# Attention scores in blocks of 128 rows, in parts of three and two blocks, in place of six blocks of 96

## The reference

```python
def _attn_ref(q, k, v):                       # (8, 8, 576, 64): batch, head, row, dim
    k_p = k.reshape(B, H, Sp, 8, D).mean(axis=3)    # 72 keys in place of 576
    v_p = v.reshape(B, H, Sp, 8, D).mean(axis=3)
    scores = scale * np.matmul(q, k_p.transpose(0, 1, 3, 2))
    scores = scores - np.max(scores, axis=-1, keepdims=True)
    attn = np.exp(scores)
    attn = attn / (np.sum(attn, axis=-1, keepdims=True) + 1e-09)
    return np.matmul(attn, v_p).astype(np.float32)

x = attn_out.transpose(0, 2, 1, 3).reshape(4608, 512)
h = x @ w_in;  x = np.maximum(0.01 * h, h) @ w_out          # layer 1, (512, 2048), (2048, 512)
h = x @ w2_in; x = h * np.clip(h + 3, 0, 6) / 6 @ w2_out    # layer 2, same sizes
```

## Time and profile before

| | |
|---|---|
| time, median of 3 runs | 1733.42 us (1729.87 to 1739.12) |
| the profiled execution's own time | 1732.34 us |
| its span in the trace | 1730.6 us |
| mean granted TensorE clock | 0.992 of full |
| instructions | 33189 |
| PE, DVE, ACT, POOL busy | 98%, 59%, 37%, 23% of the span |
| moved by DMA | 366.83 MB, 212 GB/s mean |

### The profile page before, as it was taken

The page is one execution under the profiler, slowest core; times in us unless marked ns, Lnnn a source line. Parts: engine busy times, 40 slices in busy tenths (PEclk is TensorE's granted clock), DMA queues, the critical chain, the costliest instruction groups (busy, mean ns, idle before and its releaser), DMA issues. The chain is left out here.

```text
span 1730.6 us, 33189 instructions
## 1 busy us (share of the span) xinstructions
PE 1691.3 (98%) x10588; PEld 1506.7 (87%) x10588; DVE 1024.0 (59%) x1807; ACT 632.5 (37%) x1329; POOL 394.1 (23%) x427
## 2 busy tenths in 40 slices
PE   7999999999999999999999999999999999999999
PEld 6788888988888888899999888989898888989898
DVE  7767776686766867666454655454544444444444
ACT  4554443333333433333222333333333333333332
POOL 6226542021120212103332202121211112121200
PEclk8999999999999999999999999999999999999999
DMA  7756877667676676767777757575757675757562
GB/s 199 228 159 201 271 249 247 214 201 259 204 243 220 208 247 215 242 196 268 239 258 245 257 172 224 176 220 175 218 170 220 178 219 171 223 173 223 173 197 77
DMA packets 215810, 366.83 MB, mean 212 GB/s; under 512 B 22464, under 2 KB 47040, under 8 KB 215744
## 3 DMA queue, kind: packets, MB, share of 16 engines
q1 hardware_dynamic: 215744, 366.04, 67.3%
HBM read 308.28 MB, written 57.67 MB: 211 GB/s over the span
## 5 line engine op out<-in xcount | busy, mean ns | idle before, releaser
L1416 PE MATMUL ps_h<-xs_hi,ring 128*128 128x256 f32 x3808 | 823.8, 285 | 20.5 <-ACT p L1045 15.9
L1416 PEld LDWEIGHTS ps_h<-xs_hi,ring 128*128 128x128 f32 x3808 | 645.5, 190 | 69.5 <-ACT p L1045 19.8
L1416 PE MATMUL ps_h<-xs_lo,ring 128*128 128x256 f32 x1904 | 537.4, 282 | 0.0
L1416 PEld LDWEIGHTS ps_h<-xs_lo,ring 128*128 128x128 f32 x1904 | 361.2, 190 | 27.0
L931 ACT ACTIVATE g_hi<-gate 128x512 fp32r<-128x512 f32 x288 | 181.9, 632 | 404.6 <-DVE gate L1126 221.8
L1185 DVE TENSOR_TENSOR u<-ps_h,p 128x256 f32<-128x256 f32 x272 | 114.2, 420 | 205.9 <-PE ps_h L1416 155.0
L1369 PE MATMUL ps_y<-g_hi,wout_hi 128*128 128x512 f32 x576 | 229.2, 398 | 0.5 <-DVE y_stage L1181 0.3
L1370 PE MATMUL ps_y<-g_lo,wout_hi 128*128 128x512 f32 x576 | 228.7, 397 | 0.0
L1370 PE MATMUL ps_y<-wout_lo,g_hi 128*128 128x512 f32 x576 | 227.8, 395 | 0.0
L1369 PE MATMUL ps_y<-wout_hi,g_hi 128*128 128x512 f32 x576 | 227.5, 395 | 0.1
L1371 PE MATMUL ps_y<-g_hi,wout_lo 128*128 128x512 f32 x576 | 226.1, 393 | 0.0
(11 more groups left out here) (115 smaller groups left out, 2021.4 us busy)
## 6 DMA issues: line engine op xcount, KB each, us to landing
ring<-w_in_split SPq DMA_DIRECT2D x920, 256.0 KB, 2.8
w_in_split<-ring SPq DMA_DIRECT2D x56, 256.0 KB, 3.6
w_in_split<-stage SPq DMA_DIRECT2D x56, 256.0 KB, 4.3
k_raw<-in_kT SPq DMA_DIRECT2D x32, 288.0 KB, 3.4
q_raw<-in_qT SPq DMA_DIRECT2D x32, 288.0 KB, 3.1
v_raw<-in_v SPq DMA_DIRECT2D x32, 288.0 KB
x0T<-x_stage SPq DMA_DIRECT2D x32, 288.0 KB, 4.4
x1T<-y_stage SPq DMA_DIRECT2D x36, 256.0 KB, 3.8
```

The costliest lines, as they stand in the source:

```text
L1416: mm = pe.matmul(banks[BANK_OF[r]], a, b[:, r, c, :], start=r in OPENS and c == 0 and n == 0, stop=c == 1 and n == 2, skip_group_check=True)
```

## The change

The six blocks of 96 rows become five of 128. The first part has the blocks at rows 0, 128 and 256; the second those at 384 and 448. The last two overlap by 64 rows, which are scored and normalized again; of the last block only its rows 64 to 127 are transposed (`AGAIN`). So a unit has 5 score matmuls (weights 128 x 128), passes of 128 partitions x 432 and 128 x 288 on DVE and ACT, 10 transposes (8 of 128 rows and 2 of 64), and products of 384 columns in `pv0` and of 192 in `pv1`. `units[0]` gets two buffers for q, used by turns, and its q load waits for the scores of the unit before the last. The x0 loads of tiles 1 to 6 move from places 18, 30 and 42 to 20, 32 and 44, those of tile 0 likewise by two, and the loads of tile 0 come one or two places earlier. `gap` is resized so that later buffers keep their places. The diff, with context and like edits left out:

```diff
@@ -15,10 +15,13 @@
-ROWS = 96
-SUB = S // ROWS
-HALF_SUB = SUB // 2
-HALF = S // 2
+BLOCK_AT = ((0, P, 2 * P), (3 * P, S - P))
+PART_BEGINS = (0, 3 * P)
+PART_QUERIES = (3 * P, S - 3 * P)
+SLOTS = (slice(0, 6), slice(6, 10))
+AGAIN = 4 * P - (S - P)
@@ -49,15 +52,15 @@
-X_PLACES = (18, 30, 42, 53)
+X_PLACES = (20, 32, 44, 53)
-FIRST_LOAD_PLACES = (6, 19, 30, 41)
+FIRST_LOAD_PLACES = (4, 18, 29, 40)
-FIRST_X_PLACES = (22, 33, 44, 54)
+FIRST_X_PLACES = (24, 35, 46, 54)
@@ -159,22 +162,23 @@
-            u.q_raw = buf("q_raw", [P, 2, HALF])
+            u.q_raw = [buf(f"q_raw{i}_", [P, S]) for i in range(1 if c else 2)]
-                buf("gap", [P, 4 * HALF + PAIR_KEYS])
+                buf("gap", [P, 2 * S + PAIR_KEYS - 240])
-            u.prob = buf("prob", [ROWS, 2, HALF_SUB * 2, KEYS])
-            u.row_max = buf("row_max", [ROWS, 2, HALF_SUB * 2])
-            u.pT_hi = buf("pT_hi", [KEYS, 2, HALF], F32R)
-            u.x0_stage = buf("x0_stage", [P, 2, HALF])
+            u.prob = buf("prob", [P, 10, KEYS])
+            u.row_max = buf("row_max", [P, 12])
+            u.pT_hi = buf("pT_hi", [KEYS, 2, PART_QUERIES[0]], F32R)
+            u.x0_stage = buf("x0_stage", [P, S])
...
@@ -229,6 +233,9 @@
+        def q_of(b, c):
+            return buffers(b, c).q_raw[0 if first(b) else c % 2]
@@ -382,8 +389,10 @@
-                above_zero(sp, scores_done, 2 * freed(b, c))
-                sp.dma_start(u.q_raw[:], qT[b, c]).then_inc(q_loaded[c], 16)
+                if not first(b):
+                    sp.wait_ge(scores_done, 2 * (freed(b, c) - 1))
+                sp.dma_start(q_of(b, c)[:], qT[b, c]).then_inc(q_loaded[c], 16)
@@ -534,7 +542,7 @@
-            sp.dma_start(units[0].q_raw[:], qT[1, 0]).then_inc(q_loaded[0], 16)
+            sp.dma_start(q_of(1, 0)[:], qT[1, 0]).then_inc(q_loaded[0], 16)
@@ -955,13 +963,14 @@
-                        nc.scalar.activation(u.prob[:, half], u.prob[:, half], ACT.Exp,
-                                             scale=SCORE_SCALE).then_inc(exp_ready, 1)
+                        nc.scalar.activation(u.prob[:, SLOTS[half]], u.prob[:, SLOTS[half]],
+                                             ACT.Exp, scale=SCORE_SCALE).then_inc(exp_ready, 1)
-                    nc.scalar.activation(u.pT_hi[:], u.ps[0:KEYS, :, 0:HALF], ACT.Copy
+                    n_q = PART_QUERIES[half]
+                    nc.scalar.activation(u.pT_hi[:, :, 0:n_q], u.ps[0:KEYS, :, 0:n_q], ACT.Copy
@@ -969,8 +978,10 @@
-                    nc.scalar.activation(u.x0_stage[:, half, :], u.ps[:, half, 0:HALF],
-                                         ACT.Copy, scale=V_SCALE).then_inc(x0_copied, 1)
+                    begins, n_q = PART_BEGINS[half], PART_QUERIES[half]
+                    nc.scalar.activation(u.x0_stage[:, begins:begins + n_q],
+                                         u.ps[:, half, 0:n_q], ACT.Copy, scale=V_SCALE
+                                         ).then_inc(x0_copied, 1)
@@ -1206,34 +1218,37 @@
-                        nc.vector.tensor_reduce(u.row_max[:, half], scores(u, half), AXIS_X,
+                        nc.vector.tensor_reduce(u.row_max[:, SLOTS[half]], scores(u, half), AXIS_X,
-                        nc.vector.tensor_tensor(u.prob[:, half], scores(u, half),
-                                                spread(u.row_max[:, half]), ALU.subtract
+                        nc.vector.tensor_tensor(u.prob[:, SLOTS[half]], scores(u, half),
+                                                spread(u.row_max, half), ALU.subtract
-                        nc.vector.tensor_reduce(u.row_sum[:, half], u.prob[:, half], AXIS_X,
-                                                ALU.add).then_inc(sum_ready, 1)
...
-                    dve.wait_ge(pT_hi_ready, 2 * n + int(name[-1]) + 1)
-                    nc.vector.tensor_tensor(u.pT_lo[:], u.ps[0:KEYS, :, 0:HALF],
-                                            u.pT_hi[:].bitcast(F32), ALU.subtract
+                    half = int(name[-1])
+                    n_q = PART_QUERIES[half]
+                    dve.wait_ge(pT_hi_ready, 2 * n + half + 1)
+                    nc.vector.tensor_tensor(u.pT_lo[:, :, 0:n_q], u.ps[0:KEYS, :, 0:n_q],
+                                            u.pT_hi[:, :, 0:n_q].bitcast(F32), ALU.subtract
@@ -1449,10 +1464,10 @@
-                        for at in range(HALF_SUB):
+                        for at, begins in enumerate(BLOCK_AT[half]):
-                                u.ps[0:ROWS, half, at * PAIR_KEYS:(at + 1) * PAIR_KEYS],
-                                u.q_raw[:, half, at * ROWS:(at + 1) * ROWS], u.kT[:],
+                                u.ps[:, half, at * PAIR_KEYS:(at + 1) * PAIR_KEYS],
+                                q_of(b, c)[:, begins:begins + P], u.kT[:],
@@ -1461,10 +1476,13 @@
-                        for j in range(HALF_SUB):
-                            mm = pe.transpose(u.ps[0:KEYS, hd, j * ROWS:(j + 1) * ROWS],
-                                              u.prob[:, half, 2 * j + hd, :],
-                                              ident[0:ROWS, 0:ROWS])
+                        for j, begins in enumerate(BLOCK_AT[half]):
+                            rows = slice(AGAIN if begins == S - P else 0, P)
+                            to = begins + rows.start - PART_BEGINS[half]
+                            mm = pe.transpose(
+                                u.ps[0:KEYS, hd, to:to + P - rows.start],
+                                u.prob[rows, SLOTS[half].start + 2 * j + hd, :],
+                                ident[rows, rows])
@@ -1472,8 +1490,10 @@
-                        mm = product(u.ps[:, half, 0:HALF], (u.v_hi[:, hd, :], u.v_lo[:, hd, :]),
-                                     (u.pT_hi[:, hd, :], u.pT_lo[:, hd, :]), hd == 0, hd == 1)
+                        n_q = PART_QUERIES[half]
+                        mm = product(u.ps[:, half, 0:n_q], (u.v_hi[:, hd, :], u.v_lo[:, hd, :]),
+                                     (u.pT_hi[:, hd, 0:n_q], u.pT_lo[:, hd, 0:n_q]),
+                                     hd == 0, hd == 1)
```

More of the change, by code:

```diff
@@ L166, in attention_buffers @@
             if c:
-                buf("gap", [P, 4 * HALF + PAIR_KEYS])
+                buf("gap", [P, 2 * S + PAIR_KEYS - 240])
             u.v_hi = buf("v_hi", [KEYS, 2, P], F32R)
             u.v_lo = buf("v_lo", [KEYS, 2, P], F32R)
-            u.prob = buf("prob", [ROWS, 2, HALF_SUB * 2, KEYS])
-            u.row_max = buf("row_max", [ROWS, 2, HALF_SUB * 2])
-            u.row_sum = buf("row_sum", [ROWS, 2, HALF_SUB * 2])
-            u.row_den = buf("row_den", [ROWS, 2, HALF_SUB * 2])
-            u.row_inv = buf("row_inv", [ROWS, 2, HALF_SUB * 2])
-            u.pT_hi = buf("pT_hi", [KEYS, 2, HALF], F32R)
-            u.pT_lo = buf("pT_lo", [KEYS, 2, HALF], F32R)
-            u.x0_stage = buf("x0_stage", [P, 2, HALF])
+            u.prob = buf("prob", [P, 10, KEYS])
+            u.row_max = buf("row_max", [P, 12])
+            u.row_sum = buf("row_sum", [P, 12])
+            u.row_den = buf("row_den", [P, 12])
+            u.row_inv = buf("row_inv", [P, 12])
+            u.pT_hi = buf("pT_hi", [KEYS, 2, PART_QUERIES[0]], F32R)
+            u.pT_lo = buf("pT_lo", [KEYS, 2, PART_QUERIES[0]], F32R)
+            u.x0_stage = buf("x0_stage", [P, S])
             return u
@@ L324, in first_chunk @@
         def first_chunk(c):
-            return units[c].x0_stage[:].rearrange("p a n -> p (a n)")[:, 0:N]
+            return units[c].x0_stage[:, 0:N]
         def ring_slot(q):
@@ L398, in store_x0 @@
                 sp.dma_start(x0T[c * P:(c + 1) * P, bass.ds(b * S, S)],
-                             buffers(b, c).x0_stage[:].rearrange("p a n -> p (a n)")
-                             ).then_inc(x0_stored[c], 16)
+                             buffers(b, c).x0_stage[:]).then_inc(x0_stored[c], 16)
             def load_x(src, col, c):
@@ L1185, in add, with spread @@
                 return nc.vector.tensor_tensor(to, banks[bank], other, ALU.add)
-            def spread(per_row):
-                return per_row.unsqueeze(2).to_broadcast([ROWS, HALF_SUB * 2, KEYS])
+            def spread(per_row, half):
+                return per_row[:, SLOTS[half]].unsqueeze(2).to_broadcast(
+                    [P, 2 * len(BLOCK_AT[half]), KEYS])
             def scores(u, half):
-                return u.ps[0:ROWS, half, 0:HALF_SUB * PAIR_KEYS].rearrange(
+                return u.ps[:, half, 0:len(BLOCK_AT[half]) * PAIR_KEYS].rearrange(
                     "p (r k) -> p r k", k=KEYS)
@@ L1219, in stage @@
                         dve.wait_ge(exp_ready, 2 * n + half + 1)
-                        nc.vector.tensor_reduce(u.row_sum[:, half], u.prob[:, half], AXIS_X,
-                                                ALU.add).then_inc(sum_ready, 1)
+                        nc.vector.tensor_reduce(u.row_sum[:, SLOTS[half]],
+                                                u.prob[:, SLOTS[half]], AXIS_X, ALU.add
```

(14 more changed lines are left out.)

## The result

The kernel after takes 1705.4 us (median of 4 runs, 1704.5 to 1706.9) against 1734.1 before (4 runs): ratio 0.983, 95% interval 0.981 to 0.986, about 28.7 us less. The forecast was 1708, range 1698 to 1730. The sum came out by luck: two of its terms were wrong in size and sign, one large term was missing, and their errors cancel. The profiled execution has a span of 1702.8 us, 27.8 less than before.

A forecast was written before the change was run, and what follows sets the result against it. PE, busy 98% of the span, was taken to bound the kernel; 10.5 + 6.8 + 6.8 + 0 - 3.4 + 1.0 + 3.5 = 25.2 us saved gave 1708 us, range 1698 to 1730.

The forecast's parts named there:

- Stalls: PE's five waits on ACT's `p` in tiles 2 to 6, 13.1 us: earlier stage stores were to save 10.5 us.
- the one read from SP's queue: SP stands at place 15's q load from 277.70 to 281.11, delaying x0 store, x0 load and first stage store.
- the first rival's condition: Stalls stay if the x0 store lands after PE's place 20, so all queues as before; about 1724, chance 0.22.
- Clock: PE's clock drops behind four of the five stalls in tiles 2 to 6 were to go, saving 6.8 us.
- Scores: Score matmuls on PE: 10 f32 passes in place of 12 at 0.122 us, 6.8 us saved in 28 units.
- Transposes: PE's transposes, ten in place of twelve a unit: the same by columns, 4.6 us less by instructions; taken as 0.
- Products with v: Six matmuls of 384 columns and six of 192 replace twelve of 288 on PE, costing 3.4 us in all.
- The estimate of 107 ns: The Trainium skill's time for a 128-wide weight load; by it narrow products with v run at their weights' pace.
- The rival of the f32 rate: Narrow fp32r products in pv1 take 0.325 us each, 36.3 us more in 28 units; about 1746, chance 0.15.
- the case of a slower kernel: Narrow products with v slow enough to give about 1746 us; a measurement above 1742.1 counts as slower, chance 0.13.
- Waits in tiles 0 and 1: PE's waits on the divide and `pT_lo`, 3.1 us in tiles 0 and 1: net 1.0 us saved.
- Prologue: DVE's softmax passes from 7.7 to 36 us shrink by a sixth: 3.5 us saved, between 1 and 8.

The follow-up runs named there:

- the guard's run: The kernel before with only the two q buffers and their later guard, x0 loads at their old places: ratio 0.989, 18.5 us less.
- the padded kernel before: The kernel before with 960 unused bytes a partition ahead of xs_hi, nothing else changed: ratio 0.992, 1721.9 us.
- the kernel with the series: The kernel after with a series of fp32r matmuls and transposes of several sizes added at the end of PE's work; no total time given.
- the two pads: Unused bytes a partition ahead of xs_hi: 960 on the kernel before, ratio 0.992, 1721.9 us; 64 on the kernel after, ratio 0.991, 1720.5 us.

## Why the prediction was right in its sum and wrong in its terms

In us saved; a minus is a cost.

- *Stalls* (forecast 10.5, bounds 0 to 13.1): 13.1. The cause was the one read from SP's queue, as the guard's run shows, but two links of the chain were off. The x0 store leaves 4.4 to 5.1 us ahead of the place 20 transposes, where it was 2.2 to 2.9: 2.2 us earlier, not 3.5. And it landed 0.1 to 1.1 us behind the start of these transposes in four of the five tiles, which is the first rival's condition. In tile 2 SP stood at the x0 load until 291.76, yet the ring load behind it, which waits for PE, left only at 292.71, so the stage store lost next to nothing; in the worst tile it left 0.25 us later than in this one. The store left 2.1 us behind the transposes for the 2.0 forecast; what I undervalued was the landing: by the end of ACT's wait in tile 2 it took 3.8 us, not 4.8. The choice of 10.5 was too careful.
- *Clock* (6.8): 6.8; no fall behind the prologue.
- *Scores* (6.8): ten passes are 1.39 us where twelve were 1.63; from start to the next matmul 1.13 against 1.37 (from 260.45 to 261.82 before), on average 0.25 a unit, so 7.1 in 28 units.

```profile
261.82 0.37 PE L1416 MATMUL ps_h<-xs_hi,ring 128*128 128x256 f32 x1
```

```profile
263.07 1.39 PE L1468 MATMUL ps_att<-kT,q_raw 128*128 128x144 f32 x10
264.20 0.38 PE L1431 MATMUL ps_h<-xs_hi,ring 128*128 128x256 f32 x1
```

- *Transposes* (0, bounds 0 to 4.6): this step failed. I laid columns against instructions and didn't ask what a transpose out of rows 64 to 127 does to the weight load behind it. The forecast also charged 0.99 us a unit to the kernel before, with 0.083 for each; but the matmul behind the sixth starts 0.03 us after it, so two sixes are 0.88. After it is 0.57 and 0.79: 0.48 us a unit more, 13.4 in 28. What costs is the turn between a transpose of all rows and one of the upper half: four whole ones take 0.35 in place of 0.79, and 11.5 us come back.
- *Products with v* (-3.4): the floor is 0.112 us for the 0.109 taken. By the pace of all of them, twelve at 0.135 before against six at 0.177 and six at 0.109 on average, a unit costs 0.09 us more, -2.6. The estimate of 107 ns that the prediction sets against this part in fact bears it out. The rival of the f32 rate (0.325) is refuted, and with it the case of a slower kernel.
- *Waits in tiles 0 and 1* (1.0): 3.1 us became 2.3.
- *Prologue* (3.5): failed, -0.4 in this pair. Over more traces it is nothing either way: tile 0's first product starts at 43.7 to 47.0 us in six traces with blocks of 96, at 43.4 to 47.9 in six with blocks of 128 in parts of 384 and 192, and the mean is 45.2 in both. DVE's groups there, 7.5 to 36 us (busy us, mean ns, idle before), answer to the earlier trace rows:

```profile
L1243 DVE TENSOR_TENSOR prob<-prob,row_inv 128x432 f32<-128x432 f32 (+1 forms) x8 | 5.8, 770 | 0.1
L1236 DVE TENSOR_SCALAR row_den<-row_sum 128x10 f32<-128x10 f32 x4 | 2.6, 658 | 0.1
L1250 DVE TENSOR_TENSOR pT_lo<-ps_h,pT_hi 72x768 fp32r<-72x768 f32 (+1 forms) x2 | 1.5, 749 | 0.8 <-ACT pT_hi L973 0.8
L1250 DVE TENSOR_TENSOR pT_lo<-ps_att,pT_hi 72x768 fp32r<-72x768 f32 (+1 forms) x2 | 1.5, 748 | 1.3 <-ACT pT_hi L973 1.3
```

The passes did shrink. DVE's idle time before `pT_lo` went from 0.8 to 2.9 us (there is a third such row with 0.8); it is 0.7 to 2.6 in the six traces with blocks of 96 and 2.1 to 5.8 in the six with blocks of 128, and the first turn's chain over ACT is a third longer. So a part of the gain turned into new waits on the same engine. The divides fell from 8.3 to 5.8 (means of 1076 and 770 ns), and the tiny `row_den`, four instructions, rose from 0.8 to 2.6 (192 and 658 ns). That pair of changes isn't shown to be work of the blocks: the padded kernel before, with blocks of 96, has means of 800 and 709 ns, and the kernel with the series, with blocks of 128, 1074 and 204. That GpSimd beside it is what stretches now the divide and now `row_den` is only argued.
- *Missing*: the place of xs and xp, 13 to 15 us by the two pads. No row of before could show it; only a second kernel does.

The error of the sum was so small because +14 (place) and +2.6 (stalls) stood against -13.4 (transposes) and -3.9 (prologue). Terms as measured: 13.1 + 6.8 + 7.1 - 2.6 + 0.8 - 0.4 - 13.4 + 14 = 25.4, against 27.8 in the spans; 2 us are unassigned, within what the intervals of these runs leave open.

## What to carry to other kernels

When an engine waits on its neighbour, follow the chain into the DMA queue's own timeline: a guard on one load (0.34 us to issue) held up a store six places later and cost 19 us. Before costing work by its columns, ask which rows of the array each instruction uses and what the weight load behind it must wait for. And compare stages that a change doesn't touch: if they move too, buffers have moved, and that part of the gain can be had, or lost, with unused bytes alone: 960 brought it, 64 took it away.

## What the runs showed of the hardware

- The place of a buffer by 64 bytes changed the pace of 512-column fp32r products from 0.232 to 0.227 us, though these products read none of the moved buffers, and layer 2 tiles by 1 us. The 256-column ones, which read xs, went from 0.119 to 0.118. Multiples of 128 were the slow ones, in five kernels (177408, 179712 and, with 64 bytes more than after, 180736), 64 beside them the fast ones, in eight. Which of xs_hi, xs_lo, xp_hi and xp_lo it is, what reads it in that time, and other distances were not tried; the mechanism stays open.
- Transposes of 128 rows and of the upper 64 by turns: 0.234 and 0.176 us apart, against 0.109 and 0.056 in series of one kind; the weight load behind each turn starts late. Around a turn between rows 0 to 63 and rows 64 to 127 starts are 7 to 49 ns apart: no such wait.
- An fp32r matmul with 128-wide weights is issued no faster than every 0.112 us, with 64-wide ones 0.058.
- In the prologue PE was idle for about 3.4 us of 9 (24 to 33 us, before) ahead of the clock's fall to 1.2 GHz at 33 us; with 23 idle matmuls more in the gaps of the prologue's second half (blocks of 128) it stayed at 2.4 to the end, in all four runs.
